# Linear attention, two MLPs and a DFT on one core: the first sequence in three units of 256 tokens, chunk buffers as a ring

## The reference

```
# gated linear attention, per head, for t in 0..767
state = alpha[t][:, None] * state + outer(k[t], v[t])      # 48 x 48
y[t]  = q[t] @ state
# first MLP, per token, on x = y with the heads side by side (384 channels)
xn = (x - mean) / sqrt(var + 1e-6) * g
x  = x + relu(xn @ w_ch1) @ w_ch2                          # 384 -> 1536 -> 384
# second stage
u   = x + real(fft over tokens, then over channels)
out = u + relu(norm(u) @ w_ch1') @ w_ch2'
```

## Time and profile before

| | us |
|---|---|
| median of 3 runs (802.97 to 804.04) | 803.88 |
| the profiled execution, its own time | 795.24 |
| its span, first to last instruction | 793.7 |
| TensorE matmuls busy in the span | 781.3 |
| VectorE busy | 455.1 |
| ScalarE busy | 218.2 |
| GpSimd busy | 71.6 |
| start of the first MLP matmul of unit 0 | 34.03 |

### The profile page before, as it was taken

The page is one execution under the profiler, slowest core; times in us unless marked ns, Lnnn a source line. Parts: engine busy times, 40 slices in busy tenths (PEclk is TensorE's granted clock), DMA queues, the critical chain, the costliest instruction groups (busy, mean ns, idle before and its releaser), DMA issues.

```text
span 793.7 us, 13264 instructions
## 1 busy us (share of the span) xinstructions
PE 781.3 (98%) x5134; PEld 770.2 (97%) x5134; DVE 455.1 (57%) x1007; ACT 218.2 (27%) x414; POOL 71.6 (9%) x119
## 2 busy tenths in 40 slices
PE   7899999999999999999999999999999999999998
PEld 6899999999999999999999999999999999999998
DVE  7894756747747567477387775436543564342422
ACT  4553132132312311323234332212221222111211
POOL 2223000000000000000001300210012000300000
DMA  9726041042051320431313511130002100000000
GB/s 194 195 81 174 31 105 31 32 106 53 21 115 37 105 70 31 125 91 60 130 56 109 185 66 51 44 100 31 1 31 71 59 0 10 20 0 31 1 31 31
DMA packets 62290, 53.84 MB, mean 68 GB/s; under 512 B 26524, under 2 KB 61980, under 8 KB 62236
## 3 DMA queue, kind: packets, MB, share of 16 engines
q1 hardware_dynamic: 62236, 53.10, 23.7%
HBM read 43.65 MB, written 13.37 MB: 72 GB/s over the span
## 4 chain that ended last, share of the span: by engine, by line
PE 89%; issue 4%; DVE 4%; POOL 1%; ACT 1%; DMA 0%; POOLq 0%; DVEq 0%
PE h L46 12%; PE h L48 12%; PE h L47 12%; PE acc L46 12%; PE acc L48 12%; PE acc L47 12%; PE side_bank L1335 4%; PE side_bank L1299 3%; PE side_bank L1331 2%; PE side_bank L1313 2%; PE side_bank L1343 2%; PE side_bank L47 2%; PE side_bank L48 2%; PE side_bank L46 1%; PE side_bank L1284 1%
## 5 line engine op out<-in xcount | busy, mean ns | idle before, releaser
L123 DVE SCALAR_TENSOR_TENSOR hT_low<-h,hT_high 128x384 fp32r<-128x384 f32 x192 | 106.6, 555 | 187.5 <-ACT hT_high L118 187.3
L46 PE MATMUL h<-xnT_high,w_high 128*128 128x384 f32 x576 | 199.0, 345 | 0.9 <-DVE hT_low L123 0.6
L46 PE MATMUL acc<-w_high,hT_high 128*128 128x384 f32 x576 | 194.0, 337 | 0.3 <-DVE hT_low L123 0.3
L48 PE MATMUL h<-xnT_high,w_low 128*128 128x384 f32 x576 | 193.4, 336 | 0.0
L47 PE MATMUL h<-xnT_low,w_high 128*128 128x384 f32 x576 | 193.2, 335 | 0.0
L48 PE MATMUL acc<-w_high,hT_low 128*128 128x384 f32 x576 | 193.0, 335 | 0.0
L47 PE MATMUL acc<-w_low,hT_high 128*128 128x384 f32 x576 | 192.7, 334 | 0.0
L118 ACT ACTIVATE hT_high<-h 128x384 fp32r<-128x384 f32 x192 | 94.2, 491 | 354.1 <-PE h L48 353.8
L46 PEld LDWEIGHTS h<-xnT_high,w_high 128*128 128x128 f32 x576 | 108.4, 188 | 3.8 <-DVE hT_low L123 0.8
L46 PEld LDWEIGHTS acc<-w_high,hT_high 128*128 128x128 f32 x576 | 108.2, 188 | 0.6 <-issue 0.6
L47 PEld LDWEIGHTS h<-xnT_low,w_high 128*128 128x128 f32 x576 | 108.5, 188 | 0.0
(11 more groups left out here) (121 smaller groups left out, 805.3 us busy)
## 6 DMA issues: line engine op xcount, KB each, us to landing
stage<-w_dram SPq DMA_DIRECT2D x24, 384.0 KB, 3.4
a_in<-alpha_dram SPq DMA_DIRECT2D x7, 672.0 KB, 5.5
q_in<-q_dram SPq DMA_DIRECT2D x7, 672.0 KB, 7.7
k_in<-k_dram SPq DMA_DIRECT2D x7, 672.0 KB, 8.7
x_scratch<-x_unit SPq DMA_DIRECT2D x8, 576.0 KB, 3.7
v_pad<-v_dram SPq DMA_DIRECT2D x14, 288.0 KB, 4.9
xb<-x_scratch SPq DMA_DIRECT2D x4, 576.0 KB, 4.2
xb<-x_turned SPq DMA_DIRECT2D x4, 576.0 KB, 6.8
```

The lines of the kernel that those rows point to most:

```text
L46: pe.matmul(out, wh, xh, start=start, stop=False)
L48: return pe.matmul(out, wl, xh, start=False, stop=stop)
L123: dve.scalar_tensor_tensor(out=self.hT[1][:, j % H_SLOTS, :], in0=self.hps[j % H_BANKS][:, 0:UN], scalar=0.0, in1=self.hT[0][:, j % H_SLOT ...
```

## The change

The first sequence (768 tokens) goes through the first MLP in three units of two chunks (256 tokens) in place of two units of three chunks; the other sequences keep two units of 384. So there are 9 units in the first MLP, and only two chunks of attention stand ahead of unit 0. `CHUNKS` = 6. A class `Unit` holds for each unit its chunks and slots. The buffers by chunk (alpha, q, k, v, F, F_inv, q_mul, k_div) are rings of three. The Fori loops over the first MLP's units are written out.

```
+class Unit:
+    def __init__(self, n, b, c0, size, par, late=0):
+        self.n, self.b, self.c0, self.size, self.par = n, b, c0, size, par
+        self.base = CHUNKS * b + c0
+        self.cols = size * P
+        if size == UT:
+            self.scores, self.outputs = (1, 4, 7), (2, 5, 8)
+            self.q_slots, self.k_slots = {0: 1, 3: 2}, {2: 1, 4: 2}
+            self.next_slot, self.rows_slot = 8, 9
+        else:
+            self.scores, self.outputs = (2 + late, 5 + late), (3 + late, 6 + late)
+            self.q_slots, self.k_slots = {1 + late: 1}, {3 + late: 1}
+            self.next_slot, self.rows_slot = 7, 8
...
+ONE = [Unit(0, 0, 0, 2, 1), Unit(1, 0, 2, 2, 0, late=1), Unit(2, 0, 4, 2, 1)]
+ONE += [Unit(2 * b + half + 1, b, UT * half, UT, half) for b in range(1, B) for half in range(2)]
```

State increments by head, in column halves of the array; outputs with an unpadded v; the products by chunk with q and k:

```
             def increments(u, c):
...
                 for h in range(PAIRS):
-                    both = v_pad[:, c, h, :, :].rearrange("p two e -> p (two e)")
-                    both = both.rearrange("p (a e) -> p a e", e=D)[:, 0:4:3, :]
-                    op = pe.matmul(bank[BKU][0:R, h * 2 * D:(h + 1) * 2 * D], k_divT[:, h, :], both,
-                                   start=True, stop=True)
+                    for two in range(2):
+                        head = 2 * h + two
+                        op = pe.matmul(bank[BKU][HR[two], h * D:(h + 1) * D], k_divT[:, h, HR[two]],
+                                       v_in[:, s, head * D:(head + 1) * D], start=True, stop=True)
...
             def outputs(u, c):
...
-                    for two in range(2):
-                        op = pe.matmul(y, probs[two][:, h, :], v_pad[:, c, h, two, :],
-                                       start=new and two == 0, stop=two == 1)
+                for two in range(2):
+                    for h in range(PAIRS):
+                        cols = slice((2 * h + two) * D, (2 * h + two + 1) * D)
+                        op = pe.matmul(y[:, cols], probs[two][:, h, :], v_in[:, s, cols],
+                                       start=new and two == 0 and h == 0, stop=two == 1 and h == PAIRS - 1)
```

`F_end` goes; `next_state` works on each head's rows in its own instruction (four VectorE instructions on 48 x 192 for two on 112 x 384):

```
+                for two, rows in enumerate(HR):
+                    op = dve.tensor_tensor(state_sum[rows, :, :], added(rows), held[rows, :, two, :], ALU.add)
+                op.then_inc(u_read, 1)
+                dve.wait_ge(u_read, done)
+                for two, rows in enumerate(HR):
+                    op = dve.tensor_tensor(to[rows, :, two, :], state_sum[rows, :, :], decay(rows), ALU.mult)
```

In DRAM alpha, q and k lie by chunk, so that a partition's row of a chunk is 2 KB in one piece (before: four pieces of 512 bytes), and v needs one DMA, not two. The order on SP's queue:

```
-            load_first(0)
-            load_first(1)
-            sp.wait_ge(pads_filled, 1)
-            load_first_v(0)
-            load_first(2)
-            load_first_v(1)
-            load_first_v(2)
+            load_early(0)
+            load_early(1)
+            load_early_v(0)
+            load_early_v(1)
             sp.dma_start(g_col[:, :], g_cols).then_inc(g_loaded, 16)
             split.dma(sp, ONE_W[:PIECES])
-            load_qka(0, 1)
-            load_v(0, 1)
-            split.dma(sp, ONE_W[PIECES:])
+            load_early(2)
+            load_early_v(2)
+            load_again(3)
+            split.dma(sp, ONE_W[PIECES:5])
+            load_again(4)
+            split.dma(sp, ONE_W[5:9])
+            load_again(5)
+            split.dma(sp, ONE_W[9:])
```

Start-up and unit 0 on VectorE, ScalarE and TensorE:

```
             next_state(ONE[0], 0)
             split.low(dve, ONE_W[0])
             mask(ONE[0], 1)
             next_state(ONE[0], 1)
             dve.wait_ge(y_final, 1)
             first_rows(0)
             first_rows(1)
             normalise(ONE[0], x_rows(ONE[0]), xn_one, (0,))
             normalise(ONE[0], x_rows(ONE[0]), xn_one, (1,))
             for i in range(ONE[0].size):
                 for k in range(KD):
                     low_first(k, i)
             bound_chunk(2)
...
             def side_zero(j):                      # VectorE
                 if j == 0:
                     split.low(dve, ONE_W[1])
                     prepare_q(ONE[1], 0)
                 if j == 1:
                     prepare_k(ONE[1], 0)
                 if j in (2, 3):
                     dve.wait_ge(split.low_done, ONE_W[2] + 1)
                     split.low(dve, ONE_W[1 + j])
                 side_one(ONE[1], ONE[2], j)
...
             def side_zero(j):                      # ScalarE
                 if j == 0:
                     clamp(3)
                 side_one(ONE[1], j)
                 if 3 + j < len(ONE_W):
                     split.high(act, ONE_W[3 + j])
                 if j in (6, 9):
                     clamp(4 + j // 9)
...
-                keep_clock((0, 5, 4)[i])
+                keep_clock((5, 2)[i])
```

More of the change, by code:

```diff
@@ L766, in side_one @@
+            def side_one(u, slot):
+                for c in range(u.size):
+                    if slot == u.scores[c] and not u.last(c):
+                        copy_kT(u, c)
+                    if slot == u.outputs[c]:
+                        copy_y(u, c)
                 if slot == 4:
-                    check_range(n, par)
-                if slot in (2, 5, 8):
-                    copy_y(n, slot // 3, par)
+                    check_range(u)
                 for k in TRANSPOSES_ONE.get(slot, ()):
-                    high_xT(n, par, k, g_col[:, k:k + 1])
+                    high_xT(u, k, g_col[:, k:k + 1])
@@ L994, in next_state, with added, decay @@
+                def added(rows):
+                    return of_pairs(bank[BKU][rows, 0:PAIRS * D])
+                def decay(rows):
+                    return F[rows, u.slot(c), :, P - 1:P].to_broadcast([D, PAIRS, D])
                 dve.wait_ge(u_summed, done)
[L995 to L996 removed]
+                if u.new(c):
+                    for two, rows in enumerate(HR):
+                        op = dve.tensor_tensor(to[rows, :, two, :], added(rows), decay(rows), ALU.mult)
+                    op.then_inc(u_read, 1)
@@ new lines, in side_one @@
+            def side_one(u, following, slot):
+                if slot in u.scores:
+                    mask(u, u.scores.index(slot))
+                if slot in u.q_slots:
+                    prepare_q(u, u.q_slots[slot])
+                if slot in u.k_slots:
+                    prepare_k(u, u.k_slots[slot])
+                if slot in u.outputs:
+                    next_state(u, u.outputs.index(slot))
+                if slot == u.next_slot and following:
+                    if following.b > 0:
+                        bound_alpha(following)
+                    prepare_q(following, 0)
+                if slot == u.rows_slot:
+                    dve.wait_ge(y_final, u.n + 1)
+                    for i in range(u.size):
+                        dve.wait_ge(x_ready, u.base + i + 1)
+                        statistics(u, i, x_rows(u)(i))
+                if slot == u.rows_slot + 1:
+                    normalise(u, x_rows(u), xn_one)
+                if slot == 10 and following:
+                    prepare_k(following, 0)
```

884 lines of the change are left out of this document (424 added, 460 removed).

## The result

The changed kernel took 813.8 us (median of 4 runs, 810.83 to 815.26). The kernel before, run beside it, took 803.42 us (795.17 to 804.04). The ratio is 1.0149, with a 95% interval of 1.0077 to 1.0221. The forecast was 811.5 us, within 800 to 826. The profiled execution, the fastest of the four, took 810.83 us with a span of 809.3.

The account below looks back on a forecast made before the run. TensorE's matmuls, filling 98% of the span, were taken as the bound. The terms -2.3 + 0.5 + 2.4 + 5.85 + 1.2 sum to +7.65 us, put on the 803.88 us median: 811.5 us, range 800 to 826.

Parts of the forecast that it names:

- (A): The main case for the whole kernel: all terms as summed, +7.65 us, giving 811.5 us; chance 0.48.
- The base: Whole-kernel time the sum was added to: the runs' median of 803.88 us, 8.6 above the profiled execution.
- Rival (E): TensorE's clock falls: start-up and unit 0 alone cost 3 to 5 us, chance 0.10; behind each output slot, 0.05.
- Start-up: Before unit 0: first MLP matmul near 26.3 us, a net gain of 2.3 us, bounds 1 to 3.5.
- 256 columns: Sequence 0's first-MLP matmuls at 256 columns: 0.1173 us each, a loss of 0.5 us.
- Outputs: Attention output matmuls: halving columns from 96 to 48 changes nothing, since the weight load hides the streaming.
- Increments: State increments by head in column halves: 0.12 us more for each of 20 chunks, a loss of 2.4 us.
- Unit 0: First MLP unit: TensorE stalls of 6.65 us against 0.8 before, a loss of 5.85 us, bounds 2 to 10.
- The first, 2.7: Unit 0, before pe_up(2): TensorE waits 2.7 us for piece 2's low part, which hangs on piece 1's.
- The second: Unit 0, before pe_up(4): TensorE waits 1.8 us for piece 4 behind VectorE's queue.
- The third: Unit 0, before pe_up(10): piece 9's DMA, late behind load_again(5), leads to a 1.45 us wait.
- Units 1 and 2: Sequence 0's later units: VectorE late to dve_low(11) and the normalised rows, a loss of 1.2 us, bounds 0 to 2.5.

Follow-up runs that it names:

- b_same: The kernel before, unchanged, profiled: 803.11 us median of 10 runs, four at 795.09 to 795.92 and six at 803.10 to 806.23.
- b_keep: The kernel before with short idle TensorE gaps in the start-up filled by matmuls nobody reads: 795.89 us.
- a_keep: The changed kernel with unread matmuls filling TensorE's idle time in the start-up and before pe_up(2) and pe_up(4): 805.82 us.
- a_out96: The changed kernel with each head's output matmul streaming its pair's 96 columns, not its own 48: 807.45 us.
- b_out48: The kernel before with each head's output matmul streaming its own 48 columns, not the padded 96: 804.5 us.
- a_keep_queue: a_keep with weight pieces 9 to 11 issued ahead of load_again(5) on SP's queue: 802.46 us.
- a_combo: a_keep_queue plus splits of pieces 1 and 2 ahead of unit 0, second prepare_q behind piece 4's low part, less filling before pe_up(4): 799.65 us.
- b_best_fill: b_keep with increments in column halves from the second unit on, by pairs in the start-up, and more start-up gaps filled: 793.9 us.
- b_keep_halves: b_keep with state increments made head by head in column halves and state updates on each head's rows: 799.1 us.

## Why the prediction was right, and where its steps were not

The sign and the size were right, 811.5 us against 813.8. Much of that is luck: two errors of about 4 us offset each other (the increments came out 4.0 us cheaper than forecast, unit 0's stalls 4.5 us dearer), and I had not understood the base. By the prediction's own signs (A) did not hold as written either, for it said "wrong if the clock drops", and the clock dropped.

- **The base.** I put the sum on the median, 8.6 us above the profiled execution, and left that distance unexplained. It is TensorE's clock in the start-up (b_same and b_keep, without a trace of a run near 803). The changed kernel loses the clock in each of its runs, so its median stands to a run at full clock (a_keep, 805.8) as the median of before stood to 795.2: 8.0 and 8.6 us. The sum was right on that base by luck. Against the kernel before's faster runs the changed kernel is 18.6 us slower, against its slower ones some 10.
- **Rival (E)** happened, in the start-up and in unit 0, with 0.10 on it. I gave it 3 to 5 us; between the medians of the changed kernel and of a_keep it is 8.0, of which a_out96, whose clock falls in unit 0 alone, gives back 6.4. The two profiled executions lie 3.8 us apart (810.83 and 807.01). I argued that today's start-up is as sparse and keeps the pitch of 0.109; b_out48 shows that halving the outputs' columns is enough.
- **Start-up.** A first MLP matmul at 26.3 was right at the full clock (26.14 and 26.31 in a_out96 and a_keep), and 31.07 in the changed kernel because of the clock.
- **256 columns.** 0.119 us against 0.1173: 324 x 0.0017 makes 0.5 us more than forecast.
- **Outputs.** Nothing, as forecast, to 0.03 us in 312. What I left out is that the columns cost nothing in time and still count for the clock.
- **Increments.** Forecast +2.4, measured -0.08 x 20 = -1.6 us. The step that failed is taking a scaled load of 0.041 in series plus 0.22. The block took 0.595 with the gap ahead of it. The Trainium skill (TensorEngine Tiling (Array Packing), Tiling Modes) says that a change of mode drains TensorE and tiles of one mode run side by side; the 0.55 us that I worked out by it is nearer to the trace than mine. On the way back another 0.07 to 0.09 us are lost in the states behind, which I had in neither sum; that this is a drain too is my reading, and no run shows it.
- **Unit 0.** Forecast 6.65 us of stalls. The first, 2.7, came as 2.66. The second, forecast 1.8, is 1.64 behind a late start, and 2.9 at the full clock (1.3 of wait and 1.6 of filling in a_keep). The third is the step that was mis-sized. I let piece 9 be issued at 49.4 and land 4.6 us later; in a_keep, which starts unit 0 at 26.31 as forecast, it was issued at 51.0, 1.6 us late, and took 6.6 behind four activation loads on the same queue. With ScalarE's `clamp(4)` and VectorE's queue behind it, the stalls from there on, 2.1 in my walk with the last `dve_low`, came to 4.9 + 0.6. a_keep_queue took 3.4 us of it back. I also left out the waits for the normalised rows before the transposes, 0.8 us in a_keep_queue and a_combo; in a_keep the stalls ahead hide them.
- **VectorE in unit 0** was later than I walked, for one more reason. The first four scans of F beside a split on GpSimd, and the same four alone, in the timelines of VectorE and GpSimd:

```profile
34.03 2.94 DVE L981 TENSOR_TENSOR_SCAN F<-a_safe,zeros 112x128 f32<-112x128 f32 x4
...
41.82 1.36 DVE L981 TENSOR_TENSOR_SCAN F<-a_safe,zeros 112x128 f32<-112x128 f32 x4
...
34.20 1.86 POOL L228 TENSOR_TENSOR w_low<-stage,w_high 128x768 fp32r<-128x768 f32 x1 [6.51 <-DVE w_low L228]
```

  The scans beside GpSimd's 1.86 us take 1.58 us more. The Trainium skill (SBUF — State Buffer, Who interferes with whom) describes a port pair that VectorE and GpSimd share and that one instruction holds to its end; the 1.58 fits it. No run here took it apart.
- **Units 1 and 2.** 1.2 us forecast. TensorE is idle 0.0 us in unit 1 and 1.6 us in the 43 us of unit 2.

At the full clock these make, against the forecast's 7.65: -4.0 increments, +0.5 pitch, +0.4 unit 2, +1.1 second stall, +3.4 third, -0.6 for the units of 384, which without the column halves' part are 0.2 us a sequence shorter. The sum is 8.45 us; measured is 10.6. The remaining 2.2 us are not assigned. They are hardly the clock fall behind a_keep's long stall, since a_keep's two runs with a clock of 1.000 took 805.5 and 805.7 us, next to the median of 805.8.

## What to carry to other kernels

Before costing a change, look at all run times of the kernel, not at their median and one profile: two clusters 1% apart, each with its own granted clock, are something that an edit can fix or lose, here 8.0 us beside the 10.6 that the edit itself cost. Thinning matmuls in a stage where TensorE waits between them can take the clock down even where the pitch says that the columns are free; cheap matmuls in the gaps held it in nine of ten runs (b_keep) and in twelve of twelve (b_best_fill), but with thinner increments in the start-up in three of ten (b_keep_halves). And of a DMA on the critical path, count when it can be issued and the transfers issued around it on its queue, not its median time alone.

## What the runs showed of the hardware that I had not expected

- The kernel before runs at 795 or at 803 us, nothing between, with a clock of 0.999 to 1.000 or of 0.981 to 0.987. Filling gaps of its start-up removes the slower time in nine of ten runs. In b_out48, at the lower level from 16 us on, the start-up took 43.0 us instead of 34.0.
- The fall needed no long gap: the last two ahead of it in the changed kernel are 1.04 and 1.14 us. And once it is low the clock can stay low under load, for TensorE is busy in 10.5 of the 13 us from 16 to 29 at 0.51. The Trainium skill (TensorE: Matmul & The Clock Gate, HAM oscillation) tells of gaps in matmul activity. Here gaps alone don't decide it: those of b_out48 and of the kernel before are alike from 10 to 16 us, those of the changed kernel and of a_out96 to within 0.1 us from 9 to 16, and what differs is the streamed columns.
- Two 48-column halves of the array save 0.175 us in a block of four pairs of heads (sixteen float32 entries in place of eight), and about half of it is lost in the next matmuls of the whole array.
- The outputs' pitch is the same with 48 and 96 streamed columns (2.63 us against 2.62 for states and outputs).
